# Reordering the ScalarE and VectorE queues of the attention stage: exponentials, reciprocal, RMS means and normalisation

## The chip, the cores and the metric

The program runs on one core of a Trainium2 chip. The metric is the device time of one execution in microseconds (us). The kernel before has a median of 984.87 us over three runs (984.16 to 985.06).

The engines go by their names in the profile: PE is TensorE (PEld its weight load), DVE is VectorE, ACT is ScalarE, POOL is GpSimd, SP is SyncE, whose queue issues the DMAs. Each engine works its own list of instructions strictly in order and waits on semaphores.

## The reference, cut to what matters

```python
# q, k, v: (4, 8, 576, 64), f: (4, 8, 576)
scores = q @ k.T / sqrt(64)
decay = cumsum(log(clip(f)))[:, None] - cumsum(log(clip(f)))[None, :]
attn = softmax(where(causal, scores + decay, -1e9))
x = (attn @ v)                    # laid out as 2304 tokens x 512
# first feed-forward layer, d_ff = 1536
xn = x / sqrt(mean(x * x) + 1e-6) * rms_g
h = silu(xn @ w_gate) * (xn @ w_val)
x = h @ moe_w_out
# second feed-forward layer, d_ff = 2048
out = silu(x @ w_in) @ moe2_w_out
```

All arithmetic is float32. Products that need its precision are made in three passes from a rounded part ("high") and the remainder ("low") of each operand.

## The kernel before

The 32 heads are worked as 16 pairs (p = 0 to 15). An iteration p of the attention loop mixes two pairs: the scores of pair p and the rest of pair p - 1. There is one iteration p = 16 that only finishes pair 15. A pair has nine score tiles (s = 0 to 8): two heads times four row blocks of 128 queries, and one last tile with the remaining 64 queries of both heads. The order of every engine is written out by hand; there is no planner. What one iteration does on each engine:

- PE (lines 1902 to 1921): scores 0 and 1, transposes of tiles 4 and 5 of the pair before (six matmuls, line 1804), scores 2 and 3, transposes of tiles 6 and 7 (eight), the first part of probabilities times v (line 1853), transposes of the last tile (entries "t0", four, and "t1", one), scores of the last tile, the row factors (entries "r0", line 1827, and "r1", line 1831), the second part of probabilities times v, and then, of pair p itself, the transposes of tiles 2 and 3 (four) and of tiles 0 and 1 (line 1815). Entries pass through two PSUM banks in turn: an entry may be written only after the entry two before it has been copied out. So "t1" waits for DVE's copy of tile 7, and tile 2 of pair p waits for ACT's copy of "r0".
- DVE: `shift` (line 1327) adds the decay to a score tile and finds the row minimum; `take_out` (line 1339) copies transposes out, `invert` (line 1365) takes the reciprocal of nine row sums, `qk_round` (line 1300) rounds q and k of the next pair, `row_scales` copies "r1", `x_out` (line 1374) scales the output into `x_sb`.
- ACT: `exps` (line 987) makes the exponentials of a tile, `take_out` (line 997) and `row_scales` (line 1004) copy transposes out; "r0" is its part of the row scales, and `x_out` waits for it.
- POOL: `split_qk` (line 801) makes the low part of q and k of the next pair after `qk_round`, `mask_sums` (line 808) four masks, `row_sums` (line 815) adds an epsilon once all nine exponentials are done, `spread_factors` (line 823) spreads the reciprocals.

The first RMS norm is prepared under the last pairs. POOL sums the squares; in iterations 9 and 10 (`MEAN_PAIRS`) POOL splits the sums (lines 891 and 893), PE takes the mean over the channels in two halves (lines 1867 and 1868), and DVE takes each half out (`take_first_mean`, line 1353). In iteration 10 ACT makes a logarithm (`guess_log`), in iteration 11 an exponential (`guess_exp`, line 1014), and POOL refines that by Newton steps in iterations 11 to 13. Eight `normalise_x` (line 1406) on DVE scale the eight 128 x 384 parts of x of the first span. From them ACT makes four high blocks `xb_high` (line 1029: B11, B21, B12, B22), and POOL the low ones (`xb_lo`, line 900). The first product of the feed-forward layer (`plain_product(0, 0, 0)`, lines 1925 to 1927) stands in PE's list of iteration 16 right behind the transposes of tiles 4 and 5 of pair 15, and it reads B11 with its first six matmuls and B21 with the other six. The low block B11 comes before the low block B21 on POOL, and B21 before `row_sums(15)`.

The kernel's feed-forward stage (to the end, from about 186 us) is not touched.

Of the kernel before, what the change touches and what calls it, by code (L numbers as in the profile page):

```python
# [32 lines left out]
NPAIRS = BATCH * DC  # L33
# [21 lines left out]
GUESS_PAIR = 10  # L55
# [88 lines left out]
SQUARES_PAIR, SUMS_PAIRS, MEAN_PAIRS = 3, (8, 9), (9, 10)  # L144
# [83 lines left out]
def wait(eng, sem, value):  # L228

    if isinstance(value, int) and value <= 0:  # L230
        return
    eng.wait_ge(sem, value)


def build(nc, qk_t, v_p, f, w1, w2, gain, out):
# [3 lines left out]
    with ExitStack() as ctx:  # L239
# [738 lines left out]
        def _(act):  # L978
# [4 lines left out]
            def exps(p, s):  # L983

                act.wait_ge(shifted, TILES * p + s + 1)
                tile = probs[s][:, 0:WIDTH[s // 2] if s < TAIL else SEQ]
                nc.scalar.activation(tile, tile, ACT.Exp, bias=row_min[:, s:s + 1], scale=-1.0,  # L987
                                     accum_out=row_sum[:, p % 2, s:s + 1]).then_inc(exped, 1)

            def take_out(p, entry):  # L990

                if p == 0:
                    act.wait_ge(cum_out, 16)
                act.wait_ge(transposed, TURN[p, entry] + 1)
                wait(act, pv_done, pt_free(p, entry))
                from_bank, to = turn_view(p, entry)
                nc.scalar.activation(to, from_bank, ACT.Copy).then_inc(out_act, 1)
# [8 lines left out]
            def guess_log(span):  # L1006

                act.wait_ge(mean_out, 2 * span + 2)
                nc.scalar.activation(norm_tmp(span, 1), norm_tmp(span, 0), ACT.Ln).then_inc(ln_done, 1)

            def guess_exp(span):

                act.wait_ge(ln_done, span + 1)
                nc.scalar.activation(norm_tmp(span, 1), norm_tmp(span, 1), ACT.Exp, scale=-0.5).then_inc(guess_done, 1)
# [5 lines left out]
            def xb_high(x, name):  # L1020
                if x < NSPAN:
                    act.wait_ge(x_normed, normed_before(x) + 2 * (int(name[1]) if x else PLAIN_B_ORDER.index(name) + 1))
                else:
                    for c in range(2):
                        b = DC * (int(name[2]) - 1) + 2 * (int(name[1]) - 1) + c
                        act.wait_ge(evacuated[b], 2 * (x - NSPAN) + 2)
                if x > 0:
                    act.wait_ge(multiplied, made_before(CYCLES_OF[2 * x][0]))
                nc.scalar.activation(xb[:, 0, X_AT[name]], x_block(x % NSPAN, name), ACT.Copy).then_inc(xb_hi, 1)  # L1029
# [73 lines left out]
            for p in range(NPAIRS + 1):  # L1103
                here = p < NPAIRS
                if 0 < p < NPAIRS and p != GUESS_PAIR + 1:
                    exps(p, 0)
                    exps(p, 1)
                if p > 0:
                    take_out(p - 1, 4)
                if p == GUESS_PAIR + 1:  # L1110
                    exps(p, 0)
                elif 0 < p < NPAIRS:
                    exps(p, 2)
                    exps(p, 3)
                if p == NPAIRS:
                    xb_high(0, "B12")
                if p == NPAIRS - 1:
                    xb_high(0, "B11")
                if p > 0:
                    take_out(p - 1, 6)  # L1120
                if p == GUESS_PAIR + 1:
                    exps(p, 1)
                    exps(p, 2)
                    exps(p, 3)
                if p > 0:
                    take_out(p - 1, "t0")
                if here:
                    exps(p, 4)
                    exps(p, 5)
                    if p == 0:  # L1130
                        take_out(0, 2)
                        take_rest_sums()
                    exps(p, 6)
                if p == NPAIRS:
                    xb_high(0, "B22")
                if p > 0:
                    row_scales(p - 1)
                if p == NPAIRS - 1:
                    xb_high(0, "B21")
                    exps(p, 7)  # L1140
                    take_out(p, 2)
                    exps(p, 8)
                elif here:
                    exps(p, 7)
                    exps(p, 8)
                    if p > 0:
                        take_out(p, 2)
                if p == GUESS_PAIR + 1:
                    guess_exp(0)
                if p == PREP_PAIR:  # L1150
                    w_raw(0)
                if p == PREP_PAIR + 1:
                    w_raw(1)
                if p == GUESS_PAIR:
                    guess_log(0)
            def m1_copy(n, u):
                act.wait_ge(multiplied, made(n, "M1", u))
                if n > PLAIN:
                    act.wait_ge(c21_made, 2 * (n - 1 - PLAIN) + u + 1)
                else:  # L1160
                    act.wait_ge(sums_split, UNITS1)
                nc.scalar.activation(first_sum(u), product(n, "M1", u), ACT.Copy).then_inc(m1_out, 1)
# [114 lines left out]
        def _(dve):  # L1277
# [54 lines left out]
            def take_out(p, entry):  # L1332

                if p == 0:
                    dve.wait_ge(cum_out, 16)
                dve.wait_ge(transposed, TURN[p, entry] + 1)
                wait(dve, pv_done, pt_free(p, entry))
                from_bank, to = turn_view(p, entry)
                nc.vector.tensor_copy(to, from_bank).then_inc(out_dve, 1)  # L1339
# [57 lines left out]
            def normalise_x(span, c, t=None):  # L1397

                dve.wait_ge(gain_in, 16)
                if t is None:  # L1400
                    dve.wait_ge(newton, newton_before(span) + 3)
                else:
                    dve.wait_ge(early_step, 4 * t + 4)
                cols = slice(0, SPAN) if t is None else slice(t * TT, (t + 1) * TT)
                x = x_sb[:, c, span * SPAN + cols.start:span * SPAN + cols.stop]
                nc.vector.scalar_tensor_tensor(out=x, in0=x, scalar=gain_sb[:, c:c + 1], in1=norm_tmp(span, 1)[:, cols],
                                               op0=ALU.mult, op1=ALU.mult).then_inc(x_normed, 1)
# [73 lines left out]
            for p in range(NPAIRS + 1):  # L1481
                here = p < NPAIRS
                if p > 0:
                    take_out(p - 1, 3)
                    take_first(p - 1)
                if p == NPAIRS - 2:
                    normalise_x(0, 1, 0)
                if p == NPAIRS - 1:
                    normalise_x(0, 3, 0)
                if 0 < p < NPAIRS:  # L1490
                    for r in range(4):
                        shift(p, r)
                if p > 0:
                    take_out(p - 1, 5)
                if p == NPAIRS:
                    normalise_x(0, 2, 1)
                    normalise_x(0, 3, 1)
                if here:
                    shift(p, 4)
                    shift(p, 5)  # L1500
                if p > 0:
                    invert(p - 1)
                if here:
                    shift(p, 6)
                if p > 0:
                    take_out(p - 1, 7)
                if p in MEAN_PAIRS:
                    take_first_mean(MEAN_PAIRS.index(p), 0)
                if here:
                    shift(p, 7)  # L1510
                if p > 0:
                    take_out(p - 1, "t1")
                if 0 < p < NPAIRS - 1:
                    qk_round(p + 1)
                if p in MEAN_PAIRS:
                    take_first_mean(MEAN_PAIRS.index(p), 1)
                if p == NPAIRS - 1:
                    normalise_x(0, 0, 1)
                if p > 0:
                    row_scales(p - 1, "r1")  # L1520
                if here:
                    shift(p, 8)
                if p > 0:
                    x_out(p - 1, 0)
                if p == NPAIRS - 3:
                    normalise_x(0, 0, 0)
                if p == NPAIRS - 2:
                    normalise_x(0, 2, 0)
                if p == NPAIRS - 1:
                    normalise_x(0, 1, 1)  # L1530
                if p > 0:
                    x_out(p - 1, 1)

            def split_squares(span):

# [604 lines left out]
```

## Time and profile before

| | |
|---|---|
| median of three runs | 984.87 us (984.16 to 985.06) |
| profiled execution, its own time | 985.06 us |
| its span | 983.0 us |
| PE busy | 972.3 us (99%) |
| DVE busy | 648.1 us (66%) |
| ACT busy | 449.8 us (46%) |
| POOL busy | 342.5 us (35%) |

A row of the timeline gives the start in us from the span's start, the duration in us, the engine, the line, the operation, what it writes and reads, and how often it stands in a row. In square brackets is the idle time of the engine just before it and what ended that. PE's first product of the feed-forward layer starts at 176.02 us, so the stretch that the change touches is about a sixth of the span.

### The profile page before, as it was taken

To read this page: it belongs to the slowest core of one execution; us is meant where nothing else is said; L and a number is where in the kernel's file an instruction comes from. 1 tells how busy PE (TensorE), PEld (TensorE's weight loads), DVE (VectorE), ACT (ScalarE), POOL (GpSimd) and SP (SyncE) were. 2 spreads that over 40 slices of the span, in tenths; PEclk is the share of its full clock that TensorE was granted. 3 is DMA by queue.
4 is the path that set the end of the run, shared out by engine and by line. 5 is a ranking of instruction groups with operands and counts; after the bars stand their busy time and mean duration, and the time that the engine had idled before them with its cause. 6 is when DMAs were issued, how large, how long until landed. Compare 5 with 4: busy or idle time off the path is not lost.

```text
span 983.0 us, 16362 instructions
## 1 busy us (share of the span) xinstructions
PE 972.3 (99%) x5807; PEld 891.2 (91%) x5807; DVE 648.1 (66%) x1259; ACT 449.8 (46%) x961; POOL 342.5 (35%) x326
## 2 busy tenths in 40 slices
PE   8999999999999999999999999999999999999998
PEld 5777777899999999999999999989989899898996
DVE  7878889778758797788781787705837048371441
ACT  6877786545254234344242343624616236152341
POOL 6777766504202564226233243120221202212022
PEclk9999999999999999999999999999999999999999
DMA  7668565386727666579469466341573425734212
GB/s 205 200 178 246 167 192 156 97 309 235 281 108 269 255 246 234 192 263 344 169 276 330 182 260 256 139 171 76 193 257 123 173 90 193 256 114 167 106 36 93
DMA packets 74144, 192.68 MB, mean 196 GB/s; under 512 B 8464, under 2 KB 38928, under 8 KB 67920
## 3 DMA queue, kind: packets, MB, share of 16 engines
q1 hardware_dynamic: 74064, 191.64, 54.9%
q8 instruction: 47, 0.77, 0.3%
q14 instruction: 33, 0.27, 0.1%
HBM read 150.12 MB, written 41.49 MB: 195 GB/s over the span
## 4 chain that ended last, share of the span: by engine, by line
PE 82%; ACT 1%; DVE 0%; issue 0%
PE banks L1925 20%; PE banks L1926 20%; PE banks L1927 20%; PE banks L2058 7%; PE banks L2057 7%; PE banks L2056 7%; PE banks L1804 0%; PE banks L1853 0%; ACT probs L987 0%; PE banks L1756 0%; DVE scratch L1604 0%; ACT xb L1029 0%; PE banks L2032 0%; PE banks L2033 0%; DVE x_sb L1624 0%
## 5 line engine op out<-in xcount | busy, mean ns | idle before, releaser
L1925 PE MATMUL banks<-xb,wu 128*128 128x384 f32 x864 | 288.9, 334 | 0.0
L1927 PE MATMUL banks<-xb,wu 128*128 128x384 f32 x864 | 288.7, 334 | 0.0
L1926 PE MATMUL banks<-xb,wu 128*128 128x384 f32 x864 | 288.6, 334 | 0.0
L861 POOL TENSOR_TENSOR wd<-stage_d,wd 128x512 fp32r<-128x512 f32 x84 | 119.1, 1423 | 468.8 <-ACT wd L1079 468.8
L1925 PEld LDWEIGHTS banks<-xb,wu 128*128 128x128 f32 x864 | 162.2, 188 | 0.3
L1926 PEld LDWEIGHTS banks<-xb,wu 128*128 128x128 f32 x864 | 162.2, 188 | 0.2
L1927 PEld LDWEIGHTS banks<-xb,wu 128*128 128x128 f32 x864 | 162.2, 188 | 0.0
L1172 ACT ACTIVATE scratch<-scratch 128x384 f32<-128x384 f32 x144 | 75.3, 523 | 113.0 <-DVE scratch L1562 51.1
L1181 ACT ACTIVATE hid_main<-scratch 128x384 fp32r<-128x384 f32 x144 | 72.2, 517 | 118.2 <-DVE scratch L1604 118.2
L1611 DVE TENSOR_TENSOR hid_main<-scratch,hid_main 128x384 fp32r<-128x384 f32 x144 | 88.3, 627 | 40.6 <-ACT hid_main L1181 36.3
L1079 ACT ACTIVATE wd<-stage_d 128x512 fp32r<-128x512 f32 x84 | 51.6, 630 | 135.3 <-PE banks L2058 100.3
L1925 PE MATMUL banks<-hid_main,wd 128*128 128x384 f32 x288 | 96.7, 336 | 0.1
L1927 PE MATMUL banks<-hid_main,wd 128*128 128x384 f32 x288 | 96.2, 334 | 0.0
L1926 PE MATMUL banks<-hid_main,wd 128*128 128x384 f32 x288 | 96.2, 334 | 0.0
L987 ACT ACTIVATE probs<-probs,row_min 128x128 f32<-128x128 f32 (+2 forms) x144 | 82.6, 576 | 14.7 <-DVE row_min L1327 14.6
L2058 PE MATMUL banks<-wd,hid_main 128*128 128x512 f32 x216 | 84.1, 390 | 0.0
L2057 PE MATMUL banks<-wd,hid_main 128*128 128x512 f32 x216 | 84.1, 390 | 0.0
L2056 PE MATMUL banks<-wd,hid_main 128*128 128x512 f32 x216 | 84.0, 389 | 0.0
L1621 DVE COPY x_sb<-banks 128x384 f32<-128x384 f32 (+1 forms) x21 | 12.7, 613 | 103.8 <-PE banks L2058 82.9
L1624 DVE TENSOR_TENSOR x_sb<-x_sb,banks 128x384 f32<-128x384 f32 (+1 forms) x42 | 24.8, 612 | 59.4 <-PE banks L2058 50.7
L1804 PE MATMUL banks<-ident,probs 128*128 128x128 f32 x368 | 55.6, 283 | 1.8 <-DVE ptb L1339 1.6
L1925 PEld LDWEIGHTS banks<-hid_main,wd 128*128 128x128 f32 x288 | 54.0, 188 | 1.1 <-POOL wd L861 0.4
(194 smaller groups left out, 1705.2 us busy)
## 6 DMA issues: line engine op xcount, KB each, us to landing
wu<-kept SPq DMA_DIRECT2D x48, 1792.0 KB, 10.2
stage_d<-w SPq DMA_DIRECT2D x84, 256.0 KB, 2.8
kept<-ws SPq DMA_DIRECT2D x14, 1024.0 KB, 5.3
kept<-wu SPq DMA_DIRECT2D x12, 768.0 KB, 4.6
qk_raw<-qk_t SPq DMA_DIRECT2D x14, 576.0 KB, 3.4
cum_b<-cum_dram SPq DMA_DIRECT2D x30, 256.0 KB, 4.4
kept<-xb SPq DMA_DIRECT2D x6, 1024.0 KB, 5.2
kept<-ws SPq DMA_DIRECT2D x8, 768.0 KB, 5.2
```

Of the source, the lines that this page charges most:

```text
L861: nc.gpsimd.tensor_tensor(wd[:, d % 2, 1, :], stage_d[:, d % 2, :], f32(wd[:, d % 2, 0, :]), ALU.subtract).then_inc(wd_split, 1)
L987: nc.scalar.activation(tile, tile, ACT.Exp, bias=row_min[:, s:s + 1], scale=-1.0, accum_out=row_sum[:, p % 2, s:s + 1]).then_inc(exped, 1)
L1172: nc.scalar.activation(to, src, ACT.Silu).then_inc(silu_done, 1)
L1181: nc.scalar.activation(hid_of(n, u, i, 0), src, ACT.Copy).then_inc(hid_hi, 1)
L1611: nc.vector.tensor_tensor(hid_of(n, at, i, 1), plain_output(1, i) if plain(n) else output(u, i), f32(hid_of(n, at, i, 0)), ALU.subtract).t ...
L1804: last = nc.tensor.transpose(dst[:, P * k:P * (k + 1)], probs[s][:, P * j:P * (j + 1)], ident[:, :])
L1925: nc.tensor.matmul(dst, w_hi_part, m_hi, start=start, stop=False)
L1926: nc.tensor.matmul(dst, w_hi_part, m_lo, start=False, stop=False)
L1927: return nc.tensor.matmul(dst, w_lo_part, m_hi, start=False, stop=stop)
L2056: nc.tensor.matmul(dst, hi, w_hi_part, start=first, stop=False)
L2057: nc.tensor.matmul(dst, hi, w_lo_part, start=False, stop=False)
L2058: end = nc.tensor.matmul(dst, lo, w_hi_part, start=False, stop=last)
```

## The change

On ACT, `exps(p, 7)` stands before `row_scales(p - 1)` in every iteration; `guess_exp(0)` moves from the end of iteration 11 to a place before its `row_scales`; in iteration 15, B11 is made after `row_scales` and B21 at the very end. On DVE, `invert` moves behind `shift(p, 6)` in every iteration; the second `take_first_mean` of iterations 9 and 10 stands before `qk_round`; and the `normalise_x` move: two each at the end of iterations 13, 14 and 15, behind both `x_out`, and the last two in iteration 16 behind the copy of "t1". No instruction is added or taken away.

```diff
--- before.py
+++ after.py
@@ -1114,8 +1114,6 @@
                     exps(p, 3)
                 if p == NPAIRS:
                     xb_high(0, "B12")
-                if p == NPAIRS - 1:
-                    xb_high(0, "B11")
                 if p > 0:
                     take_out(p - 1, 6)
                 if p == GUESS_PAIR + 1:
@@ -1131,28 +1129,27 @@
                         take_out(0, 2)
                         take_rest_sums()
                     exps(p, 6)
+                    exps(p, 7)
                 if p == NPAIRS:
                     xb_high(0, "B22")
+                if p == GUESS_PAIR + 1:
+                    guess_exp(0)
                 if p > 0:
                     row_scales(p - 1)
                 if p == NPAIRS - 1:
-                    xb_high(0, "B21")
-                    exps(p, 7)
+                    xb_high(0, "B11")
+                if here:
+                    exps(p, 8)
+                if 0 < p < NPAIRS:
                     take_out(p, 2)
-                    exps(p, 8)
-                elif here:
-                    exps(p, 7)
-                    exps(p, 8)
-                    if p > 0:
-                        take_out(p, 2)
-                if p == GUESS_PAIR + 1:
-                    guess_exp(0)
                 if p == PREP_PAIR:
                     w_raw(0)
                 if p == PREP_PAIR + 1:
                     w_raw(1)
                 if p == GUESS_PAIR:
                     guess_log(0)
+                if p == NPAIRS - 1:
+                    xb_high(0, "B21")
             def m1_copy(n, u):
                 act.wait_ge(multiplied, made(n, "M1", u))
                 if n > PLAIN:
@@ -1483,26 +1480,17 @@
                 if p > 0:
                     take_out(p - 1, 3)
                     take_first(p - 1)
-                if p == NPAIRS - 2:
-                    normalise_x(0, 1, 0)
-                if p == NPAIRS - 1:
-                    normalise_x(0, 3, 0)
                 if 0 < p < NPAIRS:
                     for r in range(4):
                         shift(p, r)
                 if p > 0:
                     take_out(p - 1, 5)
-                if p == NPAIRS:
-                    normalise_x(0, 2, 1)
-                    normalise_x(0, 3, 1)
                 if here:
                     shift(p, 4)
                     shift(p, 5)
+                    shift(p, 6)
                 if p > 0:
                     invert(p - 1)
-                if here:
-                    shift(p, 6)
-                if p > 0:
                     take_out(p - 1, 7)
                 if p in MEAN_PAIRS:
                     take_first_mean(MEAN_PAIRS.index(p), 0)
@@ -1510,26 +1498,30 @@
                     shift(p, 7)
                 if p > 0:
                     take_out(p - 1, "t1")
+                if p in MEAN_PAIRS:
+                    take_first_mean(MEAN_PAIRS.index(p), 1)
                 if 0 < p < NPAIRS - 1:
                     qk_round(p + 1)
-                if p in MEAN_PAIRS:
-                    take_first_mean(MEAN_PAIRS.index(p), 1)
-                if p == NPAIRS - 1:
-                    normalise_x(0, 0, 1)
+                if p == NPAIRS:
+                    normalise_x(0, 2, 1)
+                    normalise_x(0, 3, 1)
                 if p > 0:
                     row_scales(p - 1, "r1")
                 if here:
                     shift(p, 8)
                 if p > 0:
                     x_out(p - 1, 0)
-                if p == NPAIRS - 3:
-                    normalise_x(0, 0, 0)
-                if p == NPAIRS - 2:
-                    normalise_x(0, 2, 0)
-                if p == NPAIRS - 1:
-                    normalise_x(0, 1, 1)
                 if p > 0:
                     x_out(p - 1, 1)
+                if p == GUESS_PAIR + 3:
+                    normalise_x(0, 0, 0)
+                    normalise_x(0, 1, 0)
+                if p == GUESS_PAIR + 4:
+                    normalise_x(0, 2, 0)
+                    normalise_x(0, 3, 0)
+                if p == GUESS_PAIR + 5:
+                    normalise_x(0, 0, 1)
+                    normalise_x(0, 1, 1)
 
             def split_squares(span):
```

## Rows read from the trace of the kernel before

**Rows 1.** Busy time (us) and count by engine, clock, DMA, iteration 12 (windows)

```profile
132.80:142.98 10.18, 10.18 (x91) 7.73 (x90) 8.51 (x29) 8.35 (x25) 7.59 (x10) 1.00 0.67 188
```

**Rows 2.** Timeline of DVE, then of PE, in iteration 12

```profile
136.39 0.21 DVE L1365 RECIPROCAL row_sum<-row_sum 128x9 f32<-128x9 f32 x1
...
136.82 0.69 DVE L1327 CUSTOM_DVE_ANT_1 probs<-banks,cum_b 128x512 f32<-128x512 f32 x1 [0.22 <-PE banks L1804]
...
137.44 0.69 DVE L1339 COPY ptb<-banks 128x512 f32<-128x512 f32 x1
...
138.33 0.38 PE L1769 MATMUL banks<-qk_hi 128*128 128x288 f32 x1
```

**Rows 3.** Timeline of DVE in iteration 16

```profile
179.46 0.20 DVE L1365 RECIPROCAL row_sum<-row_sum 128x9 f32<-128x9 f32 x1
...
179.58 0.62 DVE L1339 COPY ptb<-banks 128x512 f32<-128x512 f32 x1
```

**Rows 4.** Timeline of PE: entry t1 of iterations 4 and 6

```profile
53.70 0.30 PE L1804 MATMUL banks<-ident,probs 128*128 128x128 f32 x1 [1.01 <-DVE ptb L1339]
...
74.72 0.30 PE L1804 MATMUL banks<-ident,probs 128*128 128x128 f32 x1 [0.18 <-DVE ptb L1339]
```

**Rows 5.** Timeline of DVE in iteration 6

```profile
73.89 0.69 DVE L1339 COPY ptb<-banks 128x512 f32<-128x512 f32 x1
```

**Rows 6.** Timeline of ACT in iteration 12

```profile
140.13 0.71 ACT L987 ACTIVATE probs<-probs,row_min 128x512 f32<-128x512 f32 x1
...
140.83 0.58 ACT L1004 ACTIVATE row_scale<-banks 128x512 f32<-128x512 f32 x1
```

**Rows 7.** Timeline of DVE, then of PE, in iteration 12

```profile
141.50 0.42 DVE L1374 TENSOR_TENSOR x_sb<-banks,row_scale 128x256 f32<-128x256 f32 x1
...
142.18 0.66 PE L1804 MATMUL banks<-ident,probs 128*128 128x128 f32 x4
```

**Rows 8.** Timeline of DVE in iteration 9

```profile
106.92 0.82 DVE L1300 CAST qk_hi<-qk_raw 128x1280 fp32r<-128x1280 f32 x1
...
107.84 0.36 DVE L1353 TENSOR_SCALAR early_tmp<-banks 128x192 f32<-128x192 f32 x1
```

**Rows 9.** Timeline of PE in iterations 9 and 10

```profile
107.52 0.28 PE L1868 MATMUL banks<-early_split,mean_w 128*128 128x192 f32 x1
...
111.35 0.36 PE L1756 MATMUL banks<-qk_hi 64*128 64x192 f32 x2
...
115.44 0.33 PE L1867 MATMUL banks<-early_split,mean_w 128*128 128x192 f32 x1
```

**Rows 10.** Timeline of POOL in iterations 9 and 10

```profile
107.83 2.92 POOL L801 TENSOR_TENSOR qk_lo<-qk_raw,qk_hi 128x1280 fp32r<-128x1280 f32 x1 [2.19 <-DVE qk_hi L1300]
...
114.33 1.00 POOL L893 TENSOR_TENSOR early_split<-early_tmp,early_split 128x384 fp32r<-128x384 f32 x1
```

**Rows 11.** Timeline of ACT, then of PE, in iteration 11

```profile
132.93 0.84 ACT L1014 ACTIVATE early_tmp<-early_tmp 128x768 f32<-128x768 f32 x1
...
132.00 0.66 PE L1804 MATMUL banks<-ident,probs 128*128 128x128 f32 x4
```

**Rows 12.** Timeline of PE in iteration 14

```profile
155.50 0.45 PE L1756 MATMUL banks<-qk_hi 64*128 64x384 f32 x2 [0.58 <-DVE row_min L1327]
```

**Rows 13.** Timeline of ACT in iteration 15

```profile
172.99 0.58 ACT L1004 ACTIVATE row_scale<-banks 128x512 f32<-128x512 f32 x1
...
173.47 0.83 ACT L1029 ACTIVATE xb<-x_sb 128x768 fp32r<-128x768 f32 x1
```

**Rows 14.** Timeline of POOL in iteration 16

```profile
177.28 1.83 POOL L900 TENSOR_TENSOR xb<-x_sb,xb 128x768 fp32r<-128x768 f32 x1 [0.66 <-ACT xb L1029]
```

**Rows 15.** Timeline of DVE in iteration 16, normalise_x

```profile
177.30 2.23 DVE L1406 SCALAR_TENSOR_TENSOR x_sb<-x_sb,gain_sb,early_tmp 128x384 f32<-128x384 f32 x1
```

**Rows 16.** Timeline of PE in iteration 16

```profile
175.42 0.30 PE L1804 MATMUL banks<-ident,probs 128*128 128x128 f32 x1 [0.20 <-ACT pta L997]
...
176.02 0.42 PE L1925 MATMUL banks<-xb,wu 128*128 128x384 f32 x1
```


## The prediction

> **What bounds the kernel now.** I read the page first: PE is busy 972.3 of 983.0 us. The window over iteration 12 shows 10.18 us of PE work in 10.18 us, at full granted clock [rows 1]. So the stage is PE's own time plus the places where its queue waits, and the change can only touch the waits. Then the timeline of PE, iteration by iteration. With 12 as the measure, the others up to 15 are longer by 6.3 us in all: 0.16, 1.16, 0.33, 0.31, 0.33 and 0.23 us in 3 to 8, 0.81 and 0.66 in the mean's 9 and 10, 0.43 in 11, 0.82 and 1.08 in 14 and 15. Last, the timelines of DVE, ACT and POOL around each wait, counted from the start of the eight transposes (135.92 in iteration 12, called T8 below; it lies 10.18 us after the one before). After 186 us PE has no wait that the profile lists.
>
> **Invert behind shift 6.** In iteration 12 the reciprocal runs in a hole: shift 6 at 136.82 must wait for PE anyway. The copy of tile 7 starts at 137.44 and ends at 138.13, and "t1" follows 0.14 us later, 0.06 before the matmul at 138.33 [rows 2]. So this copy already sets PE's time. Behind shift 6 the reciprocal is in that chain. Its price is the step from reciprocal to copy in iteration 16, 179.46 to 179.58: 0.12 us [rows 3]. Bounds: 0, if it hid in a pipeline, and 0.22, its whole length with the gap that followed it in other places; I take 0.12, the same two instructions. VectorE: DVE Perf Modes, "The TRN2 errata", in the Trainium skill would make it 58 + 9 cycles, an estimate of 0.07 us; the row is longer and I keep it.
>
> In iterations 3 to 7 the reciprocal waits for POOL's `row_sums`, with shift 6 behind it, and "t1" waits for the copy: PE is idle 1.01 and 0.18 us in 4 and 6 [rows 4]. Now shift 6 goes first, at T8 + 0.90. Iteration 6 (T8 72.06): copy at 72.96 + 0.62 + 0.12 = 73.70 instead of 73.89 [rows 5], so -0.19; the same in 7, -0.20 in 5, -0.04 in 3. In 4 the reciprocal stays late (POOL) but shift 6's 0.62 leaves the chain, with 0.09 us of waiting step: -0.71. Iterations 1, 2 and 8 pay +0.12 each. Sum to iteration 8: 0.36 - 0.04 - 0.71 - 0.20 - 0.19 - 0.19 = -0.97 us.
>
> **Exps 7 before row_scales.** ACT's copy of "r0" started at 140.83, one exponential (0.70) after exps 6 [rows 6]. It moves by 0.71 to 141.54 and ends at 142.12. PE's transposes of tile 2 need it: 142.12 + 0.14 = 142.26, against 142.18 now [rows 7], 142.30 with the 0.12 above. `x_out` moves from 141.50 to 142.20, and PE's next transposes need it at 142.76 against 142.79. So both fit under the 0.12, with 0.03 us to spare. If the reciprocal cost nothing, this would still cost 0.1. Exps 8 does not move.
>
> **Mean before qk_round.** DVE's `qk_round` starts at 106.92, the second half of the mean at 107.84, which follows PE's matmul at 107.52 + 0.28 [rows 8, 9]. In the new order `qk_round` waits for that: 107.84 + 0.28 = 108.12, +1.20. Behind it on DVE are "r1", shift 8 and `x_out`, which have that time; but POOL's low part (107.83 + 2.92 = 110.75) ends at 111.95 [rows 10], and PE wanted to start scores of pair 10 at 111.35 [rows 9]: about 112.05, +0.70. The POOL chain stays 1.20 late up to the split that ends at 115.33 [rows 10], and PE's mean matmul at 115.44 already waited for exactly that [rows 9]: 0.50 more. "t1" in 10 gets 0.12 back, since it no longer waits for DVE. Iteration 10's `qk_round` is late in the same way, by 2.00 absolute; its low part had 0.23 us of slack: scores of pair 11 come 1.76 us after their old time. Bounds: 0, if PE had slack at each handover, and 2.4, both delays in full.
>
> **Guess_exp before row_scales.** This 0.84 us operation was free at 132.93, behind everything that PE waited for; PE's transposes started at 132.00 [rows 11]. Now exps 7 (0.71) and it (0.75 from start to start) both stand before "r0": from T8 of iteration 11, 4.92 + 0.71 + 0.75 = 6.38, + 0.58 + 0.14 = 7.10, against 6.68. PE being 0.7 later swallows ACT's late start after its table loads (0.3 to 0.4 us before), which is in these counts. +0.41, so 1.76 + 0.41 = +2.17 from 9 to 11. Iteration 12 +0.12.
>
> **Normalise_x in 13 and 14.** PE waits in 14 for shifts behind normalise_x (0.58 us idle at 155.50 [rows 12]), and in 15 alike. Before, one stood between the two `x_out` and one before shift 0; now both stand behind `x_out`. Two are two, and the second `x_out` is now 0.25 later: shift 0 comes 0.09 us later than before. No gain, +0.09 twice; total of 12 to 14 +0.30. Bounds: -0.8 each (both hidden) to +0.5.
>
> **The handover in iteration 15.** ACT: "r0" moves from 172.99 by exps 7 to 173.69, so B11 is made at 174.17 to 175.00 [rows 13], exps 8 at 174.91, tile 2's copy 175.67 to 176.04, B21 175.95 to 176.79. DVE: `x_out` at 174.35 and 174.69, the first normalise_x at 175.09. POOL takes B11's low part 0.08 after ACT, at 175.08. The trace shows what such a meeting does: POOL's low part ran 177.28 to 179.11 [rows 14], and a normalise_x issued at 177.30 took 2.23 us, to 179.53, 0.42 after POOL ended [rows 15], where one alone takes 0.61. So the first normalise_x ends at 175.08 + 1.84 + 0.41 = 177.33; POOL, already waiting, takes B21 to 179.17; the second ends at 179.58. Only behind both does DVE copy tile 3 of pair 15, to 179.92, and tile 5's transposes wait for that: 180.06. PE's first product starts 0.36 later (the last three of six transposes that take 0.60), 180.42 instead of 176.02 [rows 16]: +4.40. (ACT's copy alone gives 176.18 for the start of these transposes, +0.76 on 175.42 [rows 16].)
>
> SBUF — State Buffer, "SBUF: two separate sides", in the Trainium skill says that the pair of ports which VectorE and GpSimd share is locked for a whole instruction by whoever starts first. The trace agrees, 0.42 us behind POOL's end. Were the ports shared by halves, this term would be about 1.7.
>
> The two normalise_x of iteration 16 now run while POOL is free; B22 is needed 6 us after them: nothing.
>
> **Sum.** -0.97 + 2.17 + 0.30 + 4.40 = +5.9 us on the profiled execution's 985.06 (span 983.0 and 2.06 around it): 991.0; that execution lies 0.19 above the median 984.87, so 990.8. I say 990.9.
>
> **Rivals.**
> - DVE gets in first. The meeting is at 175.08 against 175.09, which my numbers can't decide. Then the first normalise_x ends at 175.70, POOL's B11 runs to 177.44, the second ends at 177.85, tile 3's copy at 178.19, the product starts at 178.69: +2.67 for 4.40, 989.2. For it: the tie. Against: my sum has POOL ahead. Chance 0.30.
> - No mutual hold: tile 3's copy ends near 176.6, but B21's low part still comes only at 178.8 and the product's second half waits: +1.7, 988.2. Against it stand the 2.23 us. 0.10.
> - Slower still: the reciprocal costs 0.21 in nine iterations, and short gaps as in 8 (0.23) fall in bad places: 992. 0.06.
> - No change: the mean's delays are hidden and half the handover is: within 2 us of 985. 0.06.
> - Faster: the two normalise_x at the end of 13 and 14 fit in before tile 3's copy, and the waits of 14 and 15 (0.65 + 0.16 and 0.64 + 0.15) go. Place: DVE between the second `x_out` and tile 3's copy; it needs 1.1 us there, and there is 0.05. With -0.97, and the terms of 9 to 11 and the handover at zero, 985.06 - 2.6 = 982.5. It decides only if that gap exists. 0.03.
>
> My case has 0.45. About 0.2% (2 us) is what can be told from no change. Faster 0.03, same 0.06, slower 0.91. The range goes from 987.6, below the case without a hold, to 992.4, above the slow variant.
>
> **What would show it.** "t1" 0.12 us later in iteration 12, and no idle at "t1" in 5 to 7 beyond that; scores of pairs 10 and 11 waiting for POOL; iteration 11's transposes waiting for ACT; tiles 4 and 5 of pair 15 waiting for DVE's tile 3 behind two normalise_x stretched to about 2 us. The first product then starts at 176.02 - 0.97 + 2.17 + 0.30 + 4.40 = 181.9 us, or 180.2 with DVE first. I am wrong about the handover if it starts before 179.5, and about the mean if iterations 9 to 11 take no more than 0.5 us extra.

## The result and the profile after

The changed kernel ran in 991.34, 992.16 and 993.61 us and once, disturbed, in 1941 us: the median of all four is 992.88 us, that of the three undisturbed ones 992.16. The kernel before has 984.51 us, now over four runs. The ratio, without the disturbed run, is 1.0081, with a 95% interval of 1.006 to 1.010: slower by 6 to 10 us, and 992.5 us by the ratio's middle, where I had said 990.9 us and at most 992.4. The profiled execution took 991.74 us, its span is 989.7 us, 6.7 above before.

Where these 6.7 us lie, read from the starts of PE's groups in both traces (us). A row runs from one group of PE's transposes to the next; "predicted" is my term for it:

```
stretch                                           before   after    diff   predicted
to the transposes of tiles 0/1 of pair 1           26.23   26.27   +0.04    -
from there to those of pair 8                      73.82   72.65   -1.17   -0.97
to those of pair 11 (mean, guess)                  32.44   34.49   +2.05   +2.17
to those of pair 15                                42.34   42.68   +0.34   +0.30
to the first product of the feed-forward stage      1.19    5.47   +4.28   +4.40
that product, until the next transposes             2.17    3.25   +1.08    none
from there to PE's last matmul                    801.05  801.11   +0.06    0
```

Every term that I had came within 0.2 us; one was not there. (The 0.12 us that I had put on iteration 1 lie in the first row, so for the second row I had -1.09.) The timelines of DVE and PE in iteration 12 of the changed kernel, where the reciprocal now stands behind shift 6:

```profile
137.78 0.69 DVE L1324 CUSTOM_DVE_ANT_1 probs<-banks,cum_b 128x512 f32<-128x512 f32 x1 [0.35 <-PE banks L1796]
...
138.40 0.21 DVE L1362 RECIPROCAL row_sum<-row_sum 128x9 f32<-128x9 f32 x1
138.52 0.63 DVE L1336 COPY ptb<-banks 128x512 f32<-128x512 f32 x1
...
139.35 0.38 PE L1761 MATMUL banks<-qk_hi 128*128 128x288 f32 x1
```

The step from reciprocal to copy is the 0.12 us of [rows 3], but the copy itself is 0.06 shorter than in [rows 2], so PE's entry "t1" is 0.07 later and not 0.12. The iteration as a whole takes 10.31 us for the 10.18 of [rows 1]; the rest comes from ACT's later copy of "r0" (e9 and e10 below take the two edits apart). In iteration 4 PE still waits, for 0.23 us, where [rows 4] had 1.01:

```profile
53.05 0.30 PE L1796 MATMUL banks<-ident,probs 128*128 128x128 f32 x1 [0.23 <-DVE ptb L1336]
```

Iterations 9 to 11, PE's waits and what stands before "r0" on ACT:

```profile
110.82 0.35 PE L1748 MATMUL banks<-qk_hi 64*128 64x192 f32 x2 [0.56 <-POOL qk_lo L801]
...
115.44 0.33 PE L1859 MATMUL banks<-early_split,mean_w 128*128 128x192 f32 x1 [0.41 <-issue]
...
132.90 0.30 PE L1796 MATMUL banks<-ident,probs 128*128 128x128 f32 x1 [0.69 <-ACT row_scale L1004]
```

```profile
131.44 0.83 ACT L1014 ACTIVATE early_tmp<-early_tmp 128x768 f32<-128x768 f32 x1
132.17 0.58 ACT L1004 ACTIVATE row_scale<-banks 128x512 f32<-128x512 f32 x1
```

None of these waits was there before. The scores of pair 10 wait for POOL's low part, and those of pair 11 do so for 0.57 us at 122.69. The mean's matmul waits for POOL's split, which ends 0.10 us before it, at 115.34 (the profile names no releaser there). Iteration 11's transposes wait for ACT behind the exponential of the guess.

The handover in iteration 15 and 16: POOL first, then DVE, then PE.

```profile
176.25 1.82 POOL L900 TENSOR_TENSOR xb<-x_sb,xb 128x768 fp32r<-128x768 f32 x1 [4.19 <-ACT xb L1029]
...
178.03 2.11 POOL L900 TENSOR_TENSOR xb<-x_sb,xb 128x768 fp32r<-128x768 f32 x1
```

```profile
176.26 2.23 DVE L1403 SCALAR_TENSOR_TENSOR x_sb<-x_sb,gain_sb,early_tmp 128x384 f32<-128x384 f32 x1
...
178.41 2.15 DVE L1403 SCALAR_TENSOR_TENSOR x_sb<-x_sb,gain_sb,early_tmp 128x384 f32<-128x384 f32 x1
180.48 0.41 DVE L1336 COPY pta<-banks 128x256 f32<-128x256 f32 x1
```

```profile
177.34 0.30 PE L1796 MATMUL banks<-ident,probs 128*128 128x128 f32 x1 [0.84 <-ACT pta L997]
...
181.04 0.87 PE L1796 MATMUL banks<-ident,probs 128*128 128x128 f32 x3 [3.18 <-DVE pta L1336]
181.56 0.67 PE L1917 MATMUL banks<-xb,wu 128*128 128x384 f32 x1
```

POOL came 0.01 us ahead of DVE, as summed. Each normalise_x lasts until 0.42 us behind the end of POOL's instruction (178.07 and 178.49, 180.14 and 180.56), and tile 3's copy stands behind both. PE is idle 3.18 us for it. Windows show what I had left out. The first row runs from the transposes of tile 4, over PE's wait, to the product; the second covers the stretch at the lower clock, the third the product. The columns are the window, its length, the busy time of PE, PEld, DVE, ACT and POOL, and last the granted clock, the DMA share and GB/s:

```profile
177.34:181.56 4.22, 1.04 (x6) 0.83 (x7) 3.88 (x4) 1.89 (x3) 3.28 (x4) 0.87 0.00 0
180.51:183.92 3.41, 2.88 (x10) 2.91 (x11) 1.39 (x5) 0.85 (x1) 2.55 (x4) 0.50 0.00 0
181.56:184.81 3.25, 3.25 (x14) 3.22 (x13) 0.68 (x2) 0.00 (x0) 2.77 (x3) 0.64 0.00 0
```

The granted clock falls at 180.5, late in the wait of 3.18 us, to 0.50 (1.2 of 2.4 GHz), and comes back at 183.9, 2.4 us into the product: a matmul row that lasts 0.42 us at 176.02 in [rows 16] lasts 0.67 at 181.56.

### The profile page after: what moved, and what is told of

It is laid out like the page before. It is cut to its first block, busy times and chain, and to the rows that moved or that the text cites. A ratio compares the mean times of both kernels' runs of the same rounds, so it can differ in the third digit from the quotient of the medians.

```text
span 989.7 us, 16362 instructions
## 1 busy us (share of the span) xinstructions
PE 975.3 (99%) x5807; PEld 892.2 (90%) x5807; DVE 643.1 (65%) x1259; ACT 449.8 (45%) x961; POOL 343.8 (35%) x326
## 4 chain that ended last, share of the span: by engine, by line
PE 91%; POOL 3%; issue 2%; DVE 1%; ACT 1%; DMA 1%; SPq 0%; DVEq 0%; POOLq 0%
PE banks L1917 20%; PE banks L1918 20%; PE banks L1919 20%; PE banks L2049 7%; PE banks L2050 7%; PE banks L2048 7%; PE banks L1796 4%; PE banks L1748 3%; PE banks L1845 3%; POOL qk_lo L801 1%; ACT probs L987 1%; POOL cum_b L808 1%; DMA cum_b<-cum_dram 1%; PE banks L1819 0%; DMA cum_dram<-zeros 0%
## 5 line engine op out<-in xcount | busy, mean ns | idle before, releaser
L1796 PEld LDWEIGHTS banks<-ident,probs 128*128 128x128 f32 x368 | 39.7, 141 | 19.4 <-issue 8.3
```

Source lines behind the costliest of these rows:

```text
L1796: last = nc.tensor.transpose(dst[:, P * k:P * (k + 1)], probs[s][:, P * j:P * (j + 1)], ident[:, :])
```

## The experiments

Changes of time below that are called traced come from one profile each, read as in the table above. The first number is the change from the transposes of tiles 0/1 of pair 1 to the start of the first product (149.79 us in the kernel before, 155.29 in the changed one). A second number, where there is one, is the change of that product itself (2.17 and 3.25 us). Ratios are to the kernel before on the same chip. The code cuts are shortened, and their comments are mine.

**e1, the handover as before.** All of the change but iteration 15:

```diff
-                if p == NPAIRS - 1:
-                    xb_high(0, "B11")          # behind row_scales; B21 last
+                if p == NPAIRS - 1:
+                    xb_high(0, "B11")          # ahead of take_out(p - 1, 6); B21, exps 7 as before
-                    normalise_x(0, 0, 1)       # both behind x_out
-                    normalise_x(0, 1, 1)
+                    normalise_x(0, 0, 1)       # ahead of row_scales r1
+                    normalise_x(0, 1, 1)       # between the two x_out
```

> The changed kernel with iteration 15 as before on ACT (B11, B21, exps 7, copy of tile 2) and with its two normalise_x as before; all else changed. If the handover is where most went (product starting 4.3 us late, then some 1.2 us of half clock), this stands near 984.5 + 1.3 = 985.8 us, the product starts near 177.3, and the granted clock stays 1.0. Rival, the loss is spread over all 16 iterations: 989 or more.

985.87 us, ratio 1.0016 (1.0006 to 1.0025). Traced +1.35 and +0.02. The edits outside iteration 15 cost 1.4 us together, the handover the rest.

The trace also shows the meeting the other way round. Here a normalise_x starts at 175.31, 0.19 us ahead of POOL, and takes its 0.60 us; it is POOL's low part that is stretched, to 2.10 us for 1.82:

```profile
175.50 2.10 POOL L900 TENSOR_TENSOR xb<-x_sb,xb 128x768 fp32r<-128x768 f32 x1 [1.67 <-ACT xb L1029]
```

**e2, the handover alone**, the same lines of ACT and DVE moved in the kernel before.

> The kernel before with only iteration 15's order changed (ACT's exps 7 and blocks, two normalise_x behind both x_out). Handover theory with clock: first product at about 176.0 + 4.3 = 180.3, then 1.2 us at half rate, total +5.5, 990.0. If the handover needs the other edits to hurt: under 987. Without the clock's part: 988.8.

989.85 us, ratio 1.0058 (1.0041 to 1.0074). Traced +4.13 to the product and +1.57 in it. The loss needs none of the other edits. Here PE waits 3.17 us, until 178.94. The last three transposes and the product behind them, most of it at half clock, are this window:

```profile
178.94:182.95 4.01, 4.01 (x15) 3.98 (x16) 3.00 (x5) 0.40 (x1) 2.40 (x2) 0.57 0.00 0
```

**e3, PE kept busy in the wait.**

```diff
+            for _ in range(26):      # between the transposes of tiles 4 and 5 of pair 15
+                nc.tensor.transpose(product(0, "C11", 0)[:, 0:P], probs[0][:, 0:P], ident[:, :])
```

> The changed kernel with 26 transposes more on PE between the transposes of tile 4 and tile 5 of pair 15, in the wait of about 3.2 us; their result is overwritten. Clock theory: the granted clock stays at 1.0, the first product takes 2.1 us and not 3.2, total 1.2 us less than the changed kernel, about 991.0, and the runs differ less from one another. Rival, the half clock is not due to the wait: it stays, and the time is the same or up to 1 us more.

989.65 us, ratio 1.0055 (1.004 to 1.007). The wait for DVE is still there, but the clock stays up:

```profile
176.44:180.45 4.01, 3.63 (x32) 3.42 (x33) 3.92 (x4) 1.77 (x3) 3.28 (x3) 1.00 0.00 0
180.45:182.62 2.17, 2.17 (x15) 2.14 (x14) 0.68 (x2) 0.12 (x1) 1.96 (x2) 1.00 0.00 0
```

The product takes 2.17 us again, traced +0.00 against +1.08, and it starts 0.20 earlier (the last three transposes run at full clock): 1.28 us in all, as expected. The median fell by more, 2.9 us from the 992.5 of the ratio, where I had expected 1.2. In the profiles a further 0.9 us lies before pair 1's transposes (25.36 against 26.27), where the two kernels don't differ; what makes that stretch longer or shorter isn't shown. The four runs lie within 1.1 us.

**e4, tile 3's copy ahead of the two normalise_x.**

```diff
                     take_first(p - 1)
+                if p == NPAIRS:
+                    normalise_x(0, 0, 1)       # no longer at the end of iteration 15
+                    normalise_x(0, 1, 1)
```

> The changed kernel with the two normalise_x of iteration 15 behind DVE's copies of tile 3 and tile 0/1. My chain (tile 3's copy behind two normalise_x that meet POOL's low parts): transposes of tile 5 wait for ACT's copy of tile 2 only, the product starts about 0.9 us late and its second half waits for B21's low part; total about 3.5 us less than the changed kernel, 989. Rival, PE waits for B11 and B21 anyway, whatever DVE does: less than 1.5 us is won.

988.22 us, ratio 1.0039 (1.0024 to 1.0054), 4.3 us under the changed kernel's 992.5 (1.0081 x 984.51). Traced +2.22 and +0.98, 3.4 us less than the changed kernel. The product has a new wait in it for B21's low part, the next thing in line:

```profile
179.88 0.44 PE L1917 MATMUL banks<-xb,wu 128*128 128x384 f32 x1 [0.72 <-POOL xb L900]
```

**e5 and e6, the handover's two halves**, each alone in the kernel before: ACT's lines of iteration 15 in e5, the two normalise_x in e6.

> The kernel before with only ACT's iteration 15 changed (exps 7 ahead of row_scales, B11 behind it, copy of tile 2 behind exps 8, B21 last). DVE's normalise_x stay. Theory: PE waits for ACT's copy of tile 2 (+0.8) and then for B21's low part, made by POOL after B11's: product's second half near 179, total +1.7, 986.3. Rival, the ACT part alone makes the whole loss: +4 or more.

986.45 us, ratio 1.0016 (1.0006 to 1.0025). Traced +1.10 and +0.68: PE waits 0.83 us for ACT's copy of tile 2, then 0.39 for B21's low part.

> The kernel before with only the two normalise_x of iteration 15 moved behind both x_out. ACT's blocks as before, so POOL's low part of B21 (174.38 to 176.30) meets the first normalise_x at about 174.9. Theory: that normalise_x ends near 176.7, the second near 177.2, tile 3's copy near 177.6, product near 178.1: +2.1, 986.6. Rival, harmless without ACT's part: within 0.5 us.

987.28 us, ratio 1.0025 (1.0015 to 1.0034). Its normalise_x and PE's wait:

```profile
174.33 1.74 DVE L1406 SCALAR_TENSOR_TENSOR x_sb<-x_sb,gain_sb,early_tmp 128x384 f32<-128x384 f32 x1
```

```profile
177.09 0.30 PE L1803 MATMUL banks<-ident,probs 128*128 128x128 f32 x1 [1.69 <-DVE pta L1339]
```

Traced +1.88 and +1.57: here PE is idle 1.69 us, and the clock fell all the same, 0.4 us behind the end of the wait. It does not do so in every run: five of the ten runs have a mean granted clock of 1.0 and 985.83 to 986.76 us, five 0.998 and 987.80 to 988.46. What decides between them isn't shown; the profile is of one of the slower five.

**e7 and e8, the mean and the guess alone.**

```diff
+                if p in MEAN_PAIRS:
+                    take_first_mean(MEAN_PAIRS.index(p), 1)
                 if 0 < p < NPAIRS - 1:
                     qk_round(p + 1)            # e7: behind the mean
-                if p in MEAN_PAIRS:
-                    take_first_mean(MEAN_PAIRS.index(p), 1)
```

> The kernel before with only the second take_first_mean of iterations 9 and 10 ahead of qk_round. Theory: POOL's low part 1.2 and 2.0 us late, scores of pairs 10 and 11 wait, iteration 11 gives 0.3 to 0.4 back (ACT was late there): +1.3 us, 985.8. Rival, slack hides it: within 0.3.

985.70 us, ratio 1.0008 (0.9999 to 1.0018): the interval reaches no change, so the sign rests on the trace. Traced +1.61. PE waits where expected, 0.56 us each before the scores of pairs 10 and 11 (at 112.06 and 123.94), for POOL's `qk_lo`.

```diff
+                if p == GUESS_PAIR + 1:
+                    guess_exp(0)               # e8: ahead of row_scales, exps 7 behind
```

> The kernel before with only guess_exp ahead of row_scales in iteration 11 (exps 7 stays behind). Theory: ACT's copy of r0 is 0.75 us later, ends 132.05, PE's transposes of tile 2 at 132.2 for 132.0: only +0.2 us. Rival, the full 0.75 shows: +0.75.

984.75 us, ratio 1.0000 (0.9991 to 1.0009). Traced +0.23. Alone it costs hardly anything. In the changed kernel, with exps 7 ahead of "r0" as well and the mean moved, PE waits 0.69 us behind it; no run has the guess and exps 7 together without the mean.

**e9 and e10, the reciprocal and exps 7 alone**, in all iterations (e10 without 15).

```diff
-                if p > 0:
-                    invert(p - 1)
                 if here:
                     shift(p, 6)
                 if p > 0:
+                    invert(p - 1)              # e9: behind shift 6
                     take_out(p - 1, 7)
```

> The kernel before with only invert behind shift 6. Theory: copy of tile 7 later by 0.12 where the reciprocal stood in a hole (t1 about 0.07 later), earlier by up to 0.8 in iteration 4 and 0.2 to 0.3 in 5 to 7. Sum over all iterations: -1.5 + 8 x 0.07 = -1.0 us, 983.6. Rival: the price in the other iterations eats it, 0 or more.

983.10 us, ratio 0.9984 (0.9975 to 0.9992): faster than before. Traced -1.40. An iteration that has nothing else takes 10.25 to 10.27 us for 10.18: 0.07 to 0.09 more.

```diff
                     exps(p, 6)
+                    if p != NPAIRS - 1:
+                        exps(p, 7)             # e10: ahead of row_scales
```

> The kernel before with only exps 7 ahead of row_scales, in iterations 0 to 14. Theory: ACT's copy of r0 ends 0.71 later and PE's transposes of tile 2 wait for it, at 6.34 for 6.26 us after T8, the next ones 0.05 more: 12 iterations at 0.1 = +1.2 us, 985.7. Rival: a part of it was slack, 0.

985.28 us, ratio 1.0011 (1.0002 to 1.0020). Traced +0.45 only: iterations that have nothing else take 10.31 us for 10.18, but in those with a late "t1" ACT's copy was not what came last. I had counted twelve. The median is 1.2 us above before, more than that. In its profile the clock falls in iteration 1, ahead of the stretch that is called traced; the windows before and in the fall:

```profile
15.00:18.84 3.84, 2.27 (x22) 1.54 (x20) 2.16 (x11) 2.36 (x10) 2.68 (x11) 1.00 1.07 347
18.84:22.25 3.41, 3.41 (x18) 2.24 (x16) 2.26 (x9) 1.00 (x3) 1.31 (x3) 0.50 1.15 297
```

PE had been busy 2.27 of 3.84 us there, in the waits of the first iteration; in the kernel before's profile the same window has 2.17 busy and no fall. Four of e10's eleven runs have a mean clock of 0.998 and 986.78 us, five 1.0 and 984.76. On the same chip one of 33 runs of the kernel before is at 0.998 (986.66 us), and 26 at 1.0 have a mean of 984.24: at clock 1.0 e10 costs 0.5 us, as traced. The edit may make that fall more frequent; eleven runs with one profile don't settle it. On the chip of e5 to e8 two of 31 runs of the kernel before are at 0.998, 986.28 and 986.94 us, where 22 at 1.0 have a mean of 984.48.

**e11 and e12, versions of my own.**

```diff
+                if p < NPAIRS - 1:
+                    row_sums(p)                # e11, POOL: ahead of the squares
                 if 0 <= p - SQUARES_PAIR < DC:
...
                 spread_factors(p)
+                if p == PREP_PAIR + 1:
+                    w_raw(1)
```

> A version of my own: the kernel before with POOL's row_sums ahead of the squares, and the second w_raw behind spread_factors. Theory: the reciprocal is never late, so the waits at t1 in 3, 5, 6, 7 go and in 4 about 0.5 of 1.14 us is left: -1.8 us, 982.7. Rival: what POOL gives back there it takes in spread_factors or split_qk, 0.

983.30 us, ratio 0.9992 (0.9983 to 1.0000), just at the edge of what can be told from no change. Traced -1.43. All waits at "t1" up to 7 are gone, but PE waits 0.7 us for POOL's low part behind the moved `w_raw`.

```diff
+                if p in (NPAIRS - 2, NPAIRS - 1):
+                    normalise_x(0, p - (NPAIRS - 3), 0)     # e12: where invert stood; invert behind tile 7's copy
+                if p == NPAIRS - 1:
+                    normalise_x(0, 3, 0)                    # ahead of row_scales r1
...
+                    normalise_x(0, 0, 1)                    # between the two x_out of 15
+                if p == NPAIRS:
+                    normalise_x(0, 1, 1)                    # behind take_first
```

> e11 with the normalise_x spread over DVE's holes: one where the reciprocal stood in 14 and 15 (the reciprocal behind tile 7's copy), one where qk_round is missing in 15, one between the x_out of 15, one in 16 behind the first copies. Theory: the waits before scores 2 and 3 of pair 15 go and those of 14 shrink by half, -1.1 us on e11: 981.6. Rival: POOL holds the new places up as well, no gain on e11.

982.71 us, ratio 0.9987 (0.9978 to 0.9996). Traced -1.95, so 0.52 on e11, where I had said 1.1: the waits before scores 2 and 3 shrink, but in 14 the late reciprocal makes PE wait for the row factors (0.17 us at "r1", for POOL).

**e13, e6 with PE kept busy** by twelve transposes, as in e3.

> e6 (only the two normalise_x of iteration 15 moved) with 12 transposes more on PE between the transposes of tiles 4 and 5 of pair 15; their result is overwritten. Clock theory: the half clock behind PE's wait is what splits e6's runs in two groups 2 us apart, and it goes: the runs stand near the lower group, 986.0, granted clock 1.0. Rival, the groups have another cause: both remain, median 987 or more.

985.97 us, ratio 1.0018 (1.0010 to 1.0027). Ten of eleven runs lie between 985.66 and 987.13 us at 0.999 or 1.0; the group around 988.1 is gone. Traced +1.78 and +0.00, for +1.88 and +1.57 in e6. One run at 0.998 has 987.26; it has no trace.

**e14, the reciprocal behind shift 6 only where it is late, with e12's normalise_x:**

```diff
+                elif p > 0 and p not in range(3, 8):
+                    invert(p - 1)
                 if here:
                     shift(p, 6)
+                if p in range(3, 8):
+                    invert(p - 1)
```

> A version of my own: invert behind shift 6 only in iterations 3 to 7, where it waits for POOL, and the normalise_x of e12; POOL as before. Theory: 1.7 us from the first (0.16 + 0.78 + 3 x 0.25), 0.5 from the second as e12 showed over e11: 984.2 - 2.2 = 982.0. Rival: the holes are worth nothing outside e12's order, 982.7 or more.

982.28 us, ratio 0.9975 (0.9965 to 0.9985): 2.2 us under the kernel before, traced -2.21. It is the lowest ratio of all, though its interval overlaps those of e9, e11 and e12.

## Why the prediction was wrong

- **Invert behind shift 6: right in sign and place, its price too high.** With exps 7, -1.17 us for -0.97 to pair 8. I had 0.12 us for the reciprocal in a calm iteration. Alone it costs 0.07 to 0.09 (e9), because the copy behind it is 0.06 shorter, and e9 gains 1.4.
- **Exps 7: right in size, wrong in role, and partly luck.** Alone it costs 0.13 us in an iteration that has nothing else (e10), and both edits together cost the same 0.13. So it does not fit under the reciprocal: it sets the price and the reciprocal fits under it. My 0.12 came out because 0.12 for the one is nearly 0.13 for the other. In the iterations with a late "t1" it was hidden, so that e10 traced +0.45 for the 1.2 that I expected.
- **Mean before qk_round and guess_exp: right**, +2.05 for +2.17. e7 shows the mean's part alone (+1.61, I had 1.76), e8 that the guess alone costs 0.2.
- **Normalise_x in 13 and 14: right in size**, +0.34 for +0.30 from 12 to 15. No run has this edit alone. One thing changed place: in 14 and 15 PE no longer waits 0.58 us in one piece before scores 2, but in shorter ones, 0.16 of them before the transposes of tile 5.
- **The handover: its length right, its price wrong.** The chain over two normalise_x held up by POOL gave +4.28 for +4.40. Each half has its own price: ACT alone +1.8 (e5, product included), DVE alone +1.9 before the clock (e6), both +4.1 (e2); e4, which takes DVE's half away, leaves +3.2. The rival in which DVE gets in first did not come, by 0.01 us: POOL leads by that in the changed kernel, in e2 and in e3. My sum could not decide such a margin, as it said; that it had this order was luck. The rival without mutual hold fell: both engines' records are stretched, DVE's where POOL is first and POOL's where DVE is (e1).
- **The failed step is the sum behind "PE's first product starts 0.36 later, 180.42 instead of 176.02: +4.40".** I priced a wait of 3.2 us at its length, and put what comes behind it at nothing without a reason. Late in it the granted clock fell, and the three transposes and most of the product ran at 1.2 GHz: 1.28 us more (e3), of which 0.20 lies in the 4.28. The four terms that I had come to 5.50 in the trace, the product to 1.08 more and the small rest to 0.10: together the 6.7. Without the fall it would have been 5.4 for my 5.9, so that small errors on the high side hid part of the missing term. The same fall fits the two groups of e6, and the slower one is gone in e13.
- **What stays open.** The runs of the changed kernel differ by 2.3 us. The one at 993.61 us has the lowest mean clock (0.997), which would fit a second fall, as in iteration 1 of e10's profile; but a run of e2 at 0.997 (989.87 us) is no slower than one at 0.998 (989.83), and of neither at 0.997 is there a trace. Nor is it shown why the fall comes in all runs of the changed kernel and e2 and in half of those of e6.

## What to carry to other kernels

A wait of TensorE costs its length and, if the granted clock falls, a second price in the matmuls behind it: look at the clock's column around every long wait, before and after; here it fell at 1.69 us and at 3.2. An instruction that is moved to where it would wait anyway is free only if nothing else stands behind it there: count what is queued, as for `qk_round` and tile 3's copy. Where one engine's late input hurts in five of sixteen iterations, move the reader only in those: e14 traces 0.29 us better than the sum of e9's gain and of e12's over e11, less than the medians can tell.

## What the runs showed of the hardware

In the changed kernel PE waited 0.84 us and then 3.18 us, and the clock fell 0.5 us before the second wait's end; in e2, with waits of 0.84 and 3.17 us, it fell 0.4 us behind the end. In e6, with waits of 0.20 and 1.69 us, it fell 0.4 us behind the end in the profile, and by the mean clocks in five of ten runs. It did not fall in the profiles of e4 (0.84 us, and 0.72 in the product) and e5 (0.83 and 0.39), whose runs are all at 0.999 or 1.0. In the four traces that have such a fall (the changed kernel, e2, e6, e10) the stretch at half clock lasted 3.41 us.

A normalise_x that met a POOL instruction already under way was recorded with 2.23, 2.15 and 1.74 us for the 0.61 it takes alone, and ended 0.41 to 0.42 us behind POOL's; where it was first (e1) it took 0.60, and POOL's took 2.10 for 1.82. Handovers from the end of one engine's record to the start of the next were steady: DVE or ACT to PE 0.14 to 0.15 us, POOL to PE 0.05 to 0.1, ACT to POOL 0.08.
